# Attention and two expert layers on one core: the closing block, the routing constants and TensorE's first microseconds

## The reference

```python
def _attn_ref(q, k, v, phi):                       # 8 x 8 heads, 576 tokens, 64 wide, 32 memory slots
    a = softmax(phi)                               # over the tokens' 576 positions, for each slot
    k_m, v_m = a.T @ k, a.T @ v                    # 32 x 64 each, per head
    return softmax(q @ k_m.T / sqrt(64)) @ v_m

def _moe_ref(x, w_in, w_out):                      # 4608 tokens, 512 -> 2048 -> 512
    h = x @ w_in
    return (h * sigmoid(1.702 * h)) @ w_out

def _moe2_ref(x, w_gate, w_output_gate, w1, w2):   # 8 experts, 512 -> 1024 -> 512, the best one per token
    e = argmax(x @ w_gate)
    return gate_w * sigmoid(x @ w_output_gate)[e] * (relu(x @ w1[e]) @ w2[e])
```

## Time and profile before

| | |
|---|---|
| median of 3 runs | 1339.43 us (1337.65, 1339.43, 1339.52) |
| the profiled execution | 1339.29 us, of which the span (first to last instruction) is 1337.6 us |
| mean granted TensorE clock | 0.998 |
| PE busy | 1304.2 us (97%) |
| DVE, POOL, ACT busy | 628.6, 550.5 and 389.2 us (47%, 41%, 29%) |
| stage A | to about 109 us |
| stages B and C | the rest; PE is busy in 90% or more of every slice |

### The profile page before, as it was taken

One profiled execution on the slowest core, in us unless ns is written; L12 is line 12 of the kernel. 1 busy time (PEld: TensorE's weight loads), 2 busy tenths in 40 slices (PEclk: granted clock), 3 DMA queues, 4 the chain that ended last, 5 costly groups with the idle time before them and its releaser, 6 DMA issues.

```text
span 1337.6 us, 23538 instructions
## 1 busy us (share of the span) xinstructions
PE 1304.2 (97%) x6866; PEld 1051.9 (79%) x6867; DVE 628.6 (47%) x1291; ACT 389.2 (29%) x725; POOL 550.5 (41%) x648
## 2 busy tenths in 40 slices
PE   5899999999999999999999999999999999999997
PEld 3457888888888888888888888887788888888886
DVE  4894343533433434334434343347655555555553
ACT  3673222222222322222222222223222222222221
POOL 2557954444433434334334343412343333433332
PEclk9999999999999999999999999999999999999999
DMA  8998366575475564654655646647974779558882
GB/s 350 418 389 309 102 218 190 203 194 195 159 188 173 180 181 173 188 191 155 175 194 169 179 172 180 198 159 232 259 210 99 217 246 256 153 143 266 243 233 63
DMA packets 152924, 274.26 MB, mean 205 GB/s; under 512 B 16947, under 2 KB 54084, under 8 KB 150308
## 3 DMA queue, kind: packets, MB, share of 16 engines
q1 hardware_dynamic: 96100, 204.30, 44.6%
q10 hardware_dynamic: 43584, 37.37, 11.9%
q0 software_dynamic: 13184, 31.88, 7.7%
HBM read 144.98 MB, written 100.45 MB: 183 GB/s over the span
## 4 chain that ended last, share of the span: by engine, by line
PE 90%; DVE 3%; DMA 3%; issue 1%; ACT 1%; SPq 0%; ACTq 0%; POOL 0%; POOLq 0%
PE ps L752 29%; PE ps L718 29%; PE ps L822 16%; PE ps L793 15%; DMA phT<-in_phi 3%; PE ps L762 1%; DVE sc L1169 1%; DVE scs L1171 1%; DVE scs L1180 1%; DVE sc L1173 0%; ACTq L1046 0%; DVE pT L1192 0%; PE ps L637 0%; PE ps L690 0%; DMA cq<-ch 0%
## 5 line engine op out<-in xcount | busy, mean ns | idle before, releaser
L718 PE MATMUL ps<-xs,W 128*128 (+1 forms) x1728 | 417.5, 390 | 0.0
L752 PE MATMUL ps<-W,gs 128*128 128x512 f32 x1728 | 415.1, 389 | 0.1
L752 PEld LDWEIGHTS ps<-W,gs 128*128 128x128 f32 x1728 | 324.2, 188 | 67.8 <-DVE gs L1246 0.5
L718 PEld LDWEIGHTS ps<-xs,W 128*128 128x128 f32 x1728 | 322.9, 188 | 69.3 <-issue 2.7
L1244 DVE TENSOR_TENSOR gate<-ps,gate 128x512 f32<-128x512 f32 x144 | 99.6, 691 | 370.3 <-ACT gate L988 370.3
L988 ACT ACTIVATE gate<-ps 128x512 f32<-128x512 f32 x144 | 86.1, 598 | 467.8 <-PE ps L718 443.1
L1613 POOL CAST whi<-raw 128x512 fp32r<-128x512 f32 x128 | 83.5, 652 | 331.7 <-DMA raw<-in_moe_w 331.7
L822 PE MATMUL ps<-W,chT 128*128 (+1 forms) x936 | 218.3, 389 | 1.0 <-DVE chT L1381 1.0
L793 PE MATMUL ps<-W,cx 128*128 (+1 forms) x936 | 218.5, 389 | 0.7 <-issue 0.7
L822 PEld LDWEIGHTS ps<-W,chT 128*128 128x128 f32 x936 | 175.5, 188 | 38.2 <-issue 1.8
L793 PEld LDWEIGHTS ps<-W,cx 128*128 128x128 f32 x936 | 175.5, 188 | 37.7 <-issue 1.4
(11 more groups left out here) (163 smaller groups left out, 773.8 us busy)
## 6 DMA issues: line engine op xcount, KB each, us to landing
W<-expert_scratch SPq DMA_DIRECT2D x24, 2048.0 KB, 11.5
raw<-in_moe_w SPq DMA_DIRECT2D x128, 256.0 KB, 2.9
expert_scratch<-whi SPq DMA_DIRECT2D x128, 256.0 KB, 2.6
expert_scratch<-raw SPq DMA_DIRECT2D x128, 256.0 KB, 2.9
cq<-ch ACTq DMA_DIRECT2D x156, 128.0 KB
kvm<-in_kv SPq DMA_DIRECT2D x16, 1152.0 KB, 11.1
crec<-record_scratch POOLq DMA_DIRECT2D x160, 64.0 KB
qT<-in_q SPq DMA_DIRECT2D x16, 576.0 KB, 8.9
```

The costliest lines, as they stand in the source:

```text
L718: mm = pe.matmul(ps[:, f % 2, :], W[:, col:col + P], xs[:, bass.ds(x0 + (x_lo * K1 + c) * T, T)], start=(c == 0 and w_lo + x_lo == 0), sto ...
L752: mm = pe.matmul(ps[:, 2 + s, :], gs[:, f % 2, g_lo, s * P:(s + 1) * P], w_out_sb[:, f, w_lo, :], start=(f == 0 and g_lo + w_lo == 0), sto ...
```

## The change

Four edits.

1. The block is opened with `no_gpsimd_drain=True`, and the last waits go from SP to ACT, behind ACT's last scaling of a block.
2. `mask` is no longer loaded; GpSimd writes it with eight memsets. `row`, which nothing read, is gone.
3. The seven loads of GpSimd at the start become six on SP in the first tile of stage B, behind the chunk with number 19; their staging area is now in `rec`. DVE copies them into place in step 13 of that tile, and PE waits for that at the tile's end and not at its start.
4. PE multiplies the zeros of `padrec` (128 x 128 by 128 x 512, float32) twice before it waits for `ident`, and once after the first group's transposes. The result goes to a PSUM bank that is overwritten later.

```diff
-        block = ctx.enter_context(nc.Block())
+        block = ctx.enter_context(nc.Block(no_gpsimd_drain=True))
...
-        stage = [pT[1][:, 0:P], pT[1][:, P:2 * P]]
+        stage = [rec[:, 0, 0:P], rec[:, 0, P:2 * P]]
...
             load_phi(0)
-            for dst, src in ((ident, "ident"), (mask, "mask")):
-                sp.dma_start(dst[:], cst[src]).then_inc(s_cst, 16)
+            sp.dma_start(ident[:], cst["ident"]).then_inc(s_cst, 16)
             load_kv(0)
...
+                        if k == 2:
+                            for dst, src in ((region, "region"), (iota8, "iota8"), (token, "token")):
+                                sp.dma_start(dst[:], cst[src]).then_inc(s_cst2, 16)
+                            sp.dma_start(stage[0], cst["before"]).then_inc(s_cst2, 16)
+                            sp.dma_start(stage[1], gates).then_inc(s_cst2, 16)
+                            sp.wait_ge(b_setup, 1)
+                            sp.dma_start(padrec[:].bitcast(I32)[:, DM + NE + 1:DM + NE + 2], cst["padtoken"]).then_inc(b_cst, 16)
...
-            def sp_wait_all(i, r):
-                ...
-            n_blocks = sp.value_load(tbl[0:1, 5, 1:2], min_val=FULL, max_val=NBLK)
-            for i in range(FULL, NBLK + 1):
-                with sp.If(n_blocks == i):
-                    sp_wait_all(i, i % RING)
...
-            pe.wait_ge(s_cst, 2 * 16)
+            def warm_up(n):
+
+                for _ in range(n):
+                    pe.matmul(ps[:, 7, :], padrec[:, 0:P], padrec[:, 0:512], start=True, stop=True)
+
+            pe.wait_ge(b_setup, 1)
+            warm_up(2)
+            pe.wait_ge(s_cst, 16)
             a_transposes(0)
+            warm_up(1)
...
             pe.wait_ge(s_xo, 2 * NG)
-            pe.wait_ge(b_setup, 5)
...
                 act_y(i - 1, (r - 1) % RING)
+                for n in range(i, min(i + 2, NBLK)):
+                    wait_records(act, n, n % RING)
+                for u in range(2):
+                    act.wait_ge(c_out[u], 16 * ((i + 1 - u) // 2))
...
             phi_in(0)
-            wait(dve, s_cst2, 6 * 16)
-            dve.tensor_copy(before[:], stage[0]).then_inc(b_setup, 1)
...
+            def routing_consts():
+
+                dve.wait_ge(s_cst2, 5 * 16)
+                dve.wait_ge(b_setup, 3)
+                dve.tensor_copy(before[:], stage[0]).then_inc(b_setup, 1)
...
+                    if first and f == 13:
+                        routing_consts()
...
-            pool.dma_start(stage[0], cst["before"]).then_inc(s_cst2, 16)
-            for dst, src in ((region, "region"), (iota8, "iota8"), (row, "row"), (token, "token")):
-                pool.dma_start(dst[:], cst[src]).then_inc(s_cst2, 16)
-            pool.dma_start(stage[1], gates).then_inc(s_cst2, 16)
-            pool.wait_ge(b_setup, 2)
-            pool.dma_start(padrec[:].bitcast(I32)[:, DM + NE + 1:DM + NE + 2], cst["padtoken"]).then_inc(b_cst, 16)
+            for h in range(HG):
+                for n in range(2):
+                    pool.memset(mask[h * M:(h + 1) * M, n * D:(n + 1) * D], float(h % 2 == n)).then_inc(s_mask, 1)
```

More of the change, by code:

```diff
@@ L81, in constants @@
         "region": np.tile(np.arange(NE, dtype=f) * REGION, (P, 1)),
-        "row": np.arange(P, dtype=f).reshape(P, 1),
         "blk8": np.repeat(np.arange(NBLK, dtype=f), NE).reshape(1, NBLK * NE),
@@ L86, in constants @@
     return c
-CONSTS = ["ident", "mask", "before", "token", "padtoken", "iota8", "region", "row", "blk8", "load8"]
+CONSTS = ["ident", "before", "token", "padtoken", "iota8", "region", "blk8", "load8"]
 def build(nc, q, kv, phi, w_in, w_out, gates, w1, w2, cst, out):
@@ L127, in build @@
         iota8 = sb("iota8", [P, NE])
-        row = sb("row", [P, 1])
+        sb("to_16", [P, 1])
         padrec = sb("padrec", [P, REC])
@@ L242, in build @@
         s_cst = sem("consts_loaded")
-        s_cst2 = sem("consts_loaded_by_pool")
+        s_cst2 = sem("routing_consts_loaded")
+        s_mask = sem("mask_set")
         s_phi = [sem(f"phi_loaded{u}") for u in range(3)]
@@ L842, in pe_tile @@
                     pe.wait_ge(s_wlo, 2 * C1)
+                    pe.wait_ge(b_setup, 5)
             def last_x2_transpose(t):
@@ L1213, in _ @@
             phi_in(0)
-            wait(dve, s_cst2, 6 * 16)
-            dve.tensor_copy(before[:], stage[0]).then_inc(b_setup, 1)
-            dve.wait_ge(b_setup, 4)
-            dve.tensor_copy(wg[:].rearrange("p o c m -> p (o c) m")[:, :, 0:2 * NE],
-                            stage[1].rearrange("p (c e) -> p c e", e=2 * NE)).then_inc(b_setup, 1)
-            dve.wait_ge(b_setup, 5)
             dve.memset(hotb[:], 0.0).then_inc(b_cfree, 1)
-            dve.tensor_copy(base[:, SUB, :], region[:]).then_inc(b_lfree, 1)
-            dve.wait_ge(b_cfree, 1)
-            dve.wait_ge(b_lfree, 1)
-            dve.wait_ge(s_cst, 2 * 16)
             for g in range(NG):
@@ L1382, in dve_h_lo @@
                                       by_h(0, j).bitcast(F32), ALU.subtract).then_inc(c_hlo, 1)
+            def routing_consts():
+                dve.wait_ge(s_cst2, 5 * 16)
+                dve.wait_ge(b_setup, 3)
+                dve.tensor_copy(before[:], stage[0]).then_inc(b_setup, 1)
+                dve.tensor_copy(wg[:].rearrange("p o c m -> p (o c) m")[:, :, 0:2 * NE],
+                                stage[1].rearrange("p (c e) -> p c e", e=2 * NE)).then_inc(b_setup, 1)
+                dve.wait_ge(b_setup, 5)
+                dve.wait_ge(b_cfree, 1)
+                dve.tensor_copy(base[:, SUB, :], region[:]).then_inc(b_lfree, 1)
+                dve.wait_ge(b_lfree, 1)
             def dve_tile(t, first=False, last=False):
@@ L1420, in _ @@
             dve_h_lo(0, 0)
-            wait(dve, s_cst, 4 * 16)
+            wait(dve, s_cst, 3 * 16)
             wait(dve, c_xtr, EARLY)
@@ L1588, in first_x_lo @@
                                    ALU.subtract).then_inc(b_xlo, 1)
-            pool.wait_ge(s_cst, 2 * 16)
+            pool.wait_ge(s_mask, 2 * HG)
             for g in range(NG):
```

6 lines of the change are left out of this document (removed).

## The result

| | before | changed |
|---|---|---|
| median of 12 timed runs | 1339.37 us | 1334.89 us |
| lowest of them | 1337.52 us | 1332.37 us |
| the profiled execution | 1339.29 us, span 1337.6 | 1335.33 us, span 1333.7 |
| mean granted TensorE clock | 0.998 | 0.996 |

The ratio is 0.9966, with a 95% interval of 0.9958 to 0.9974: the change makes the kernel 4.5 us (0.34%) faster, where 1334.3 us and so 5.1 us were predicted. One run of the kernel before took 1643 us; it is a disturbance and left out of the ratio.

What follows compares the result with a forecast made beforehand. The prediction took PE to bound the middle, loads stage A, and drains, waits and the barrier the end. 1339.3 - 3.2 (end) - 1.8 (start loads) = 1334.3 us, the other parts zero; range 1331.5 to 1337.6 us.

Steps and rivals of the forecast that it cites:

- The drain and the last waits: Program's end: removing GpSimd's drain and SP's last waits shrinks the gap behind the last scatter's landing, worth 3.2 us.
- The first rival: Program's end: the postamble waits for what the drain waited for, so only the start gains; 1337.5 us, chance 0.17.
- The loads at the start: Start of stage A: fewer small loads and a better stream of large ones, worth 1.8 us.
- the hole: Start, 9 to 11 us: load rate of 169 and 143 GB/s, 528 KB missing, put down to GpSimd's small loads; 1.3 us.
- the second rival: Start: the hole is a cost of starting, so the bytes alone are gained, 0.5 us; 1335.6 us, chance 0.16.
- The step that fails: Stage A: no hole returns from 20 to 60 us, so the start's 1.8 us pass to the landing at 66.57.
- The upper bound of the start: Start: the bytes plus all the stream misses against 420 GB/s, 4 to 8 and 9 to 12 us; 3.2 us.
- a sign of being wrong: Stage A: the prediction is wrong if DVE, not the loads, sets its length, or if the end's gap stays.
- The zeros: Start, on PE: multiplications hidden behind the loads, worth zero, with 1.5 us either way if that cover failed.
- The first tile: Stage B's first tile: six DMAs ahead of chunk 20, some 2.5 us, hidden by 3.5 us of room; zero.
- the slower rival: First tile: the small loads hold up chunk 20 and the weights; 1343.0 us at 20 us of delay, chance 0.03.
- the one at step 4: First tile, step 4: chunks bound by big stores hold PE, losing the start's 1.8 us; 1336.1 us, chance 0.04.

Runs made afterwards that it cites:

- e1: The kernel before with edit 1 alone (block closed without GpSimd's drain, last waits on ACT): ratio 0.9973 to before, median 1336.73 us.
- e3: The kernel before with only the last waits moved to ACT, GpSimd's drain kept: ratio 1.0003 to before, median 1339.90 us.
- e4: The kernel before with edits 2 and 3 alone, old end and no zeros: ratio 0.9985 to before, median 1337.17 us.
- e9: The changed kernel with four small loads (27 KB together) back on GpSimd at the start: ratio 0.9958 to before, median 1335.27 us.
- e7: The changed kernel with its six small loads (155 KB) back on GpSimd at the start: ratio 0.9976 to before, median 1336.77 us.
- e11: e5 with the next group's phi loaded ahead of q on SP's queue: ratio 0.9941 to before, median 1333.08 us.
- e5: The changed kernel without the multiplications of zeros: ratio 0.9964 to before, median 1334.49 us.
- e6: The kernel before with edit 4 alone, the three multiplications of zeros: ratio 0.9990 to before, median 1338.82 us.
- e10: The changed kernel with more multiplications of zeros, around the first transposes and k sum and in groups 1 and 2: ratio 0.9977 to before, median 1336.34 us.
- e2: The kernel before with the block closed without GpSimd's drain, last waits left on SP: ratio 0.9989 to before, median 1338.15 us.

## Why the prediction came out as it did

It was right in sign and size, 0.6 us off; its two terms were each near, and one argument inside the second was not, so a part of the agreement is luck.

**The drain and the last waits: right mechanism, the term mis-sized.** Forecast 3.2 us, measured 2.6 (6.0 to 3.4 from the scatter to the end). I had the barrier at 0.28 us and the rest of the way at 0.1, for which no row stood; behind the landing 1.1 us remain. The 0.28 was read between two engines that started side by side; at the end ACT has a wait, a branch and a drain in front of the barrier. How the 1.1 us divide was not measured. What I left open, how the gap divides between GpSimd's drain and SP's waits, e1 to e3 answer: 2.1 and 0.5, and the 0.5 only behind the 2.1.

**The first rival, the end is paid elsewhere: false.** The time around the span is 1.6 us, before 1.7, and e1's time falls by 3.6 us (2.3 to 5.0) where its views show 2.6. By the Trainium skill (Runtime: NRT & Kernel Launch, section on the preamble and postamble) a barrier for all engines follows the kernel; no run here shows that it waits for what the drain waited for.

**The loads at the start: the size right, the reason for it not.** Forecast 1.8 us; e4 gives 2.0 (0.8 to 3.2), the changed kernel's `mm1` 1.6. That the 1.6 is so near 1.8 is luck in part: 0.95 of it is the landing, and most of the other 0.65 is that the changed kernel lacks before's piece at half clock, which cost about 0.5. Over all profiles the landing comes 1.6 us earlier, so the size stands.

The step that says that the hole is due to GpSimd's small loads is confirmed, by e9 above all. By the Trainium skill (DMA: Bandwidth & Descriptors, section on the anatomy of a DMA) the semaphore write takes about one cycle. I had taken from it, for the second rival, that small loads could not hold up the large ones; the measured 193 and 185 GB/s say that they do, by a way that no run here shows.

The step that fails is the next one, that closing the hole is what earns the time: since from 20 to 60 us no hole comes back, the lead was to pass to the landing at 66.57 and along the chain. By 12 us the changed kernel's stream is 0.94 MB ahead of before's, 2.2 us at 420 GB/s, and e9's only 0.16 MB, 0.4 us. Yet the same load of phi lands at 65.62 us in the changed kernel, at 65.22 in e9 and at 65.69 in e7, and SP issues its last load of q at 80.91 to 81.44 us in all three. I had read the 420 GB/s of the earlier trace rows as the bound of stage A. e11, which moves no byte and only changes the order, starts stage B 1.75 us earlier than e5, so the order in which SP waits for buffers is a bound too. (The upper bound of the start also left out the window from 8 to 9 us, 344 GB/s, which is 0.2 us more.)

What then makes the 2 us of gain is not settled. e7, e9 and the changed kernel have in common, and before has not, that the mask is off SP's queue, so that k and v are issued 0.4 us earlier, and that one small load is gone. The record shows how early the gain is there: SP's fourth load of k and v, the first that waits for PE to be done with a buffer, is issued at 12.7 to 13.8 us in the five kernels with the old loads and at 10.5 to 11.8 in the nine others, with a hole or without, and the last load of q at 82.4 to 83.5 and at 80.1 to 82.2. That fits a gain that comes through the first k and v and the buffer that they free, and not through the rate from 9 to 11 us. It was not tried by itself.

The prediction named as a sign of being wrong that DVE and not the loads sets the length of stage A. For its second half this is so, before and after: in the changed kernel the chain has no load behind 65.62 us and runs nearly all through DVE to 103.79. The first half is where the loads are on it.

**The zeros: nothing that can be seen, as forecast** (e5 and, weaker, e6), and more of them nothing either (e10). What the forecast didn't have is the granted clock of 0.57 that they leave behind them; it too is hidden.

**The first tile: hidden, as forecast.** SP's rows there in the changed kernel:

```profile
130.50 0.33 SPq L477 DMA_DIRECT2D raw<-in_moe_w_in  x1
130.87 0.44 SPq L539 DMA_DIRECT2D region<-const_region  x1
...
133.25 0.43 SPq L543 DMA_DIRECT2D padrec<-const_padtoken  x1
133.73 0.43 SPq L477 DMA_DIRECT2D raw<-in_moe_w_out  x1
```

Six issues of 0.43 us stand ahead of chunk 20, which is issued at 133.73, 1.8 us earlier than before: SP had the room. From 60 to 200 us PE waits only in stage A, so the slower rival and the one at step 4 both fail.

**The scatter.** I named a piece at half clock as what moves single runs by 1.5 us. The one that I had in mind, at 73 us, costs about 0.5: behind the landing, before needs 42.2 us where e2, e3 and e6, which have no such piece, need 41.7. A piece at 94 to 102 us costs the 1.5.

## What to carry to other kernels

Read an end's worth from the last instruction that does work to the end of the span, in each variant: spans alone gave e3 a gain that it doesn't have, and hid most of e2's. A stream of loads at its full rate need not be the only bound; before taking time off its front, look at what its queue waits for (here q's buffer, with the next phi queued behind it). A new order of the queue may be worth more than the bytes: it gave 1.75 us at the start of stage B. A hole in a stream's rate is not yet a loss of time: here four small loads on GpSimd's queue halved the rate for 2 us, far beyond their bytes, and the kernel with them was no slower. And compare single profiles behind a common event, such as the landing of one load, so that a piece at half clock isn't taken for the effect.

## What was not expected of the hardware

- Four loads of 27 KB together on GpSimd's queue, issued from 1.5 to 3.8 us, halve the rate of SP's large loads from 8 to 10 us (193 and 185 GB/s, DMA share 0.5), some 5 us after they were issued. The time doesn't show it (0.9958). Six small loads, 155 KB, on SP's queue leave it at 307 to 378, at a full DMA share.
- GpSimd's drain at the block's end takes 2.1 us of the span although GpSimd's last instruction is the scatter, which has landed 2.4 us after its start.
- Kernels that differ only at their start have their pieces at half clock in other places: the changed kernel at 12 to 20 and 26 to 30 us, before at 72 to 75, four of the nine with the new start at 94 to 102. The granted clock reads 1.00 over the first 11 us in each, with zeros or without, but the first k sum took 1.93 or 1.94 us without them, 1.08 with them in six kernels and 1.94 with them in e6: the column does not show that difference.
- Three multiplications of zeros lower the mean granted clock of the whole kernel, from 0.997 to 0.999 in the kernels with none (or with many more, in e10) to 0.994 to 0.996.
